# Attention in front of two MoE layers: another order of GpSimd's work and of SyncE's queue, fewer and smaller moves

## The reference

```python
def _attn_ref(q, k, v):                      # 4 batches x 8 heads, seq 576, head_dim 64
    scores = np.matmul(q, k.transpose(0, 1, 3, 2)) / np.sqrt(64)
    pos = np.arange(576)
    mask = (pos[:, None] // 64) >= (pos[None, :] // 64)
    scores = np.where(mask, scores, -1e9)
    attn = np.exp(scores - np.max(scores, axis=-1, keepdims=True))
    attn = attn / (np.sum(attn, axis=-1, keepdims=True) + 1e-09)
    return np.matmul(attn, v)
def _moe_ref(x, w_in, w_out):                # 2304 tokens, 512 -> 2048 -> 512
    h = x @ w_in
    return (h * np.clip(h + 3.0, 0.0, 6.0) / 6.0) @ w_out
def _moe2_ref(x, w_in, w_out):
    h = x @ w_in
    return (h * np.tanh(np.log1p(np.exp(h)))) @ w_out
```

## Time and profile before

| | us |
|---|---|
| median of 3 runs (984.53 to 993.46) | 988.69 |
| the profiled execution, its own time | 987.67 |
| its span | 985.9 |
| PE busy | 955.1 (97%) |
| PEld busy | 851.2 (86%) |
| DVE busy | 737.2 (75%) |
| ACT busy | 643.2 (65%) |
| POOL busy | 436.7 (44%) |

### The profile page before, as it was taken

One profiled execution on the slowest core, in us unless ns is written; L12 is line 12 of the kernel. 1 busy time (PEld: TensorE's weight loads), 2 busy tenths in 40 slices (PEclk: granted clock), 3 DMA queues, 4 the chain that ended last, 5 costly groups with the idle time before them and its releaser, 6 DMA issues.

```text
span 985.9 us, 17821 instructions
## 1 busy us (share of the span) xinstructions
PE 955.1 (97%) x6028; PEld 851.2 (86%) x6028; DVE 737.2 (75%) x1404; ACT 643.2 (65%) x1431; POOL 436.7 (44%) x423
## 2 busy tenths in 40 slices
PE   7898898999999999999999999999999999999998
PEld 6787787899888889988879898898988998998886
DVE  6777787867776576879797886877877777777654
ACT  6787898956544454454436557777777777776653
POOL 7787797776847496967775680000000000000000
PEclk9999999999999999999999999999999999999999
DMA  6878889765788977697777455556555654565255
GB/s 190 226 207 224 234 238 249 217 204 166 248 286 285 325 232 259 216 319 256 252 269 259 178 180 191 196 182 228 200 190 202 220 202 170 177 248 185 92 186 193
DMA packets 86330, 216.44 MB, mean 220 GB/s; under 512 B 10720, under 2 KB 17504, under 8 KB 86240
## 3 DMA queue, kind: packets, MB, share of 16 engines
q1 hardware_dynamic: 86096, 215.01, 66.7%
q10 hardware_dynamic: 144, 0.29, 0.1%
HBM read 162.07 MB, written 39.92 MB: 205 GB/s over the span
## 4 chain that ended last, share of the span: by engine, by line
PE 81%; DMA 6%; DVE 4%; SPq 3%; POOL 2%; issue 2%; ACT 1%; ACTq 0%; POOLq 0%; DVEq 0%
PE psum L1019 37%; PE psum L902 11%; PE psum L904 11%; PE psum L903 11%; PE psum L847 4%; DMA khi<-khi 4%; PE psum L826 3%; PE psum L806 2%; PE psum L807 1%; DVE ebuf L1591 1%; DMA ext_d<-ext_made 1%; POOL klo L1738 1%; SPq L557 1%; DVE ext_made L1497 1%; DVE glo L1597 1%
## 5 line engine op out<-in xcount | busy, mean ns | idle before, releaser
L1019 PE MATMUL psum<-ghi,osplit 128*128 128x512 f32 (+1 forms) x640 | 215.9, 371 | 0.0
L902 PE MATMUL psum<-xhi,whi 128*128 128x256 f32 (+1 forms) x640 | 187.4, 293 | 2.8 <-ACT snap L1238 2.7
L904 PE MATMUL psum<-xhi,wlo 128*128 128x256 f32 (+1 forms) x640 | 186.8, 292 | 0.0
L903 PE MATMUL psum<-xlo,whi 128*128 128x256 f32 (+1 forms) x640 | 186.6, 292 | 0.0
L1019 PE MATMUL psum<-osplit,ghi 128*128 128x512 f32 x576 | 180.8, 395 | 2.1 <-DVE glo L1597 1.3
L1597 DVE SCALAR_TENSOR_TENSOR glo<-ebuf,ghi 128x512 fp32r<-128x512 f32 x144 | 126.4, 878 | 26.2 <-ACT ghi L1286 18.3
L1286 ACT ACTIVATE ghi<-ebuf 128x512 fp32r<-128x512 f32 x144 | 90.3, 627 | 68.6 <-DVE ebuf L1591 37.7
L902 PEld LDWEIGHTS psum<-xhi,whi 128*128 128x128 f32 x640 | 120.8, 189 | 15.9 <-ACT snap L1238 4.3
L1882 POOL TENSOR_TENSOR osplit<-oraw,osplit 128x512 fp32r<-128x512 f32 x80 | 115.9, 1451 | 39.9 <-ACT osplit L1205 35.8
L1019 PEld LDWEIGHTS psum<-ghi,osplit 128*128 128x128 f32 x640 | 117.9, 189 | 15.8
L903 PEld LDWEIGHTS psum<-xlo,whi 128*128 128x128 f32 x640 | 120.8, 189 | 10.6
(11 more groups left out here) (118 smaller groups left out, 2142.8 us busy)
## 6 DMA issues: line engine op xcount, KB each, us to landing
ext<-ext_d SPq DMA_DIRECT2D x56, 768.0 KB, 4.4
osplit<-o_d SPq DMA_DIRECT2D x80, 512.0 KB, 5.7
oraw<-in_w_out SPq DMA_DIRECT2D x80, 256.0 KB, 5.6
wraw<-in_w_in SPq DMA_DIRECT2D x32, 512.0 KB, 5.4
ext_d<-ext_made SPq DMA_DIRECT2D x32, 384.0 KB, 5.3
attn_t<-ostage SPq DMA_DIRECT2D x64, 144.0 KB, 2.9
qkin<-in_qk SPq DMA_DIRECT2D x30, 288.0 KB, 4.5
o_d<-staged SPq DMA_DIRECT2D x32, 256.0 KB, 5.4
```

Of the source, the lines that this page charges most:

```text
L902: pe.matmul(dst, hi, xh, start=(start and cc == 0), stop=False, skip_group_check=True)
L903: pe.matmul(dst, hi, xl, start=False, stop=False, skip_group_check=True)
L904: last = pe.matmul(dst, lo, xh, start=False, stop=(stop and cc == 1), skip_group_check=True)
L1019: last = pe.matmul(bank(Y_BANK + c, n), stat, mov, start=(first and m == 0), stop=(final and m == 2), skip_group_check=True)
```

## The change

**GpSimd**: step n now begins with q and k of head n+4, then v of head n+2 (before: n+1), then the extra pieces. In the start, the lower part of head 1's q moves from GpSimd to DVE.

**DVE** takes over the weight sum of an early job (`mix_early`) and x's sum and scaling (`add_first_x`, `scale_first_x`), inside its step: sums between the row maxima of pieces 1 and 2, the scaling ahead of the row maximum of piece 3.

**PE**: the `klo` matmul uses rows 0 to 63 of `qs` and `klo` only. It leaves out the product of the two lower parts. `move_k_lo` is gone, and PE's wait for it.

**SP**: the output is stored by one DMA of 288 KB in place of two of 144 KB, into a DRAM tensor in another layout. A chunk of x now takes four DMAs in place of three: one of output and one of row-sum inverses for each half of the rows; this holds for all blocks of the first layer. An early weight load is two DMAs of 256 KB, one in a step. The order in a step is now `move_k_hi(n+3)`, `load_qk(n+6)`, extra loads (weights, x, w_out), `move_q_hi(n+4)`, `load_v(n+3)`, `store_o(n)`, `store_rinv`. The steps of the extra pieces change as in the tables.

```diff
-    lambda b: (12 if KIND[b] == SHORT else 6) if b < NBL else 1,
-    lambda b: 0 if KIND[b] == SHORT else 6 if b < NBL else 2 if b > NBL else 1)]
+    lambda b: (16 if KIND[b] == SHORT else 8) if b < NBL else 1,
+    lambda b: 0 if KIND[b] == SHORT else 8 if b < NBL else 2 if b > NBL else 1)]
...
-EARLY_JOBS = {3: 0, 7: 1, 11: 2, 26: 3}
-EARLY_X_LOAD, NEXT_X_LOAD = {10: (0,), 11: (1,), 12: (2,), 14: (3,)}, (27, 28)
-EARLY_X_ADD, EARLY_X_SCALE, EARLY_X_MIX = (16, 17, 18, 19), (17, 18, 19, 20), 21
-EARLY_X_HI, EARLY_X_LO = (22, 23, 24), (23, 24, 25)
-EARLY_LOADS = {0: 0, 3: 1, 8: 2, 20: 3, 22: 4, 29: 5}
+EARLY_JOBS = {3: 0, 6: 1, 9: 2, 12: 3}
+NEARLY, HALVED = len(EARLY_JOBS), 6
+EARLY_LOADS = {0: (0, 0), 1: (0, 1), 2: (1, 0), 3: (1, 1), 6: (2, 0), 7: (2, 1), 9: (3, 0), 10: (3, 1),
+               18: (4, 0), 19: (4, 1), 20: (5, 0), 21: (5, 1)}
+EARLY_X_LOAD, NEXT_X_LOAD = {11: 0, 13: 1, 15: 2, 16: 3}, (26, 27, 28, 29)
+EARLY_X_ADD, EARLY_X_MIX = (17, 18, 19, 20), 21
+EARLY_X_HI, EARLY_X_LO = (21, 22, 23), (22, 23, 24)
+EARLY_O_LOAD = (22, 23, 24)
...
@@ SP @@
-                for half in range(2):
-                    sp.dma_start(attn_t[half, head * DH:(head + 1) * DH, t0:t0 + SEQ],
-                                 ostage[n % OS][half * DH:(half + 1) * DH, :]).then_inc(o_stored[n % OS], 16)
+                sp.dma_start(attn_t[n % HEADS, :, t0:t0 + SEQ], ostage[n % OS][:, :]).then_inc(o_stored[n % OS], 16)
...
-            def load_x_chunk(x, c, cols, done):
-                sp.dma_start(x[:, 0:2, :], attn_t[:, c * P:(c + 1) * P, cols].rearrange("s p t -> p s t")
-                             ).then_inc(done, 16)
-                for h in range(2):
-                    sp.dma_start(x[h * DH:(h + 1) * DH, 2, :],
+            def load_x_chunk(x, c, cols, done, sides=range(2)):
+                for h in sides:
+                    rows = slice(h * DH, (h + 1) * DH)
+                    sp.dma_start(x[rows, 0:2, :],
+                                 attn_t[2 * c + h, :, cols].rearrange("(s d) t -> d s t", s=2)).then_inc(done, 16)
+                    sp.dma_start(x[rows, 2, :],
...
             for n in range(FIRST, NHEAD):
-                if n == FIRST or 0 <= n < NHEAD - 6:
-                    load_qk(n + 6)
-                if n == -1:
-                    move_k_hi(DIRECT)
-                    move_k_lo(DIRECT)
+                if DIRECT <= n + 3 < NHEAD:
+                    move_k_hi(n + 3)
+                if n == FIRST:
+                    load_qk(3)
+                elif n == FIRST + 1:
                     load_qk(4)
                     load_qk(5)
-                elif DIRECT < n + 3 < NHEAD:
-                    move_k_lo(n + 3)
-                    move_k_hi(n + 3)
+                elif 0 <= n < NHEAD - 6:
+                    load_qk(n + 6)
+                if n in EARLY_LOADS:
+                    load_w(*EARLY_LOADS[n])
+                if n in EARLY_X_LOAD:
+                    c = EARLY_X_LOAD[n]
+                    if c == 0:
+                        attention_stored(1)
+                    load_x_chunk(xst_plain[:, c, :, :], c, slice(0, HT), x_loaded[0])
+                if n in EARLY_O_LOAD:
+                    load_o(EARLY_O_LOAD.index(n))
...
@@ PE @@
-                    pe.wait_ge(k_lo_moved[n % QK], moves(n))
...
-                    last = pe.matmul(bank(pb, w), q_tile, klo[s][:, k0:k0 + w], start=False, stop=True)
+                    last = pe.matmul(bank(pb, w), q_upper, klo[s][0:DH, k0:k0 + w], start=False, stop=True)
...
@@ DVE @@
+                low = qs[1][DH:P, 0:SEQ]
+                dve.wait_ge(q_hi, 2)
+                nc.vector.tensor_tensor(low, qkin[1][DH:P, :], low.bitcast(F32), ALU.subtract
+                                        ).then_inc(direct_q_lo[1], 1)
...
+                if n in EARLY_JOBS:
+                    mix_early(EARLY_JOBS[n])
+                if n in EARLY_X_ADD:
+                    add_first_x(EARLY_X_ADD.index(n))
                 if in_use(n + 2):
                     row_max(n + 2, 2)
                 if in_use(n + 1):
                     split_probs_lo(n + 1, 1)
+                if n in EARLY_X_ADD:
+                    scale_first_x(EARLY_X_ADD.index(n))
...
@@ GpSimd @@
-                if DIRECT <= n + 4 <= QK:
+                if DIRECT <= n + 4 < NHEAD:
                     split_qk_hi(n + 4)
                     split_qk_lo(n + 4)
-                if n + 4 == DIRECT:
-                    split_second_k_lo()
-                    split_second_q_lo()
-                if DIRECT <= n + 4 <= QK:
+                    if n + 4 == DIRECT:
+                        split_second_k_lo()
                     place_q_lo(n + 4)
-                if in_use(n + 1):
-                    split_v_hi(n + 1)
-                    split_v_lo(n + 1)
+                if in_use(n + 2):
+                    split_v_hi(n + 2)
+                    split_v_lo(n + 2)
                 if n in EARLY_JOBS:
-                    mix_early(EARLY_JOBS[n])
                     split_early_hi(EARLY_JOBS[n])
...
-                if n in EARLY_X_ADD:
-                    add_x(0, EARLY_X_ADD.index(n))
-                if n in EARLY_X_SCALE:
-                    scale_x(0, EARLY_X_SCALE.index(n))
...
-                if QK < n + 4 < NHEAD:
-                    split_qk_hi(n + 4)
-                    split_qk_lo(n + 4)
-                    place_q_lo(n + 4)
```

More of the change, by code:

```diff
@@ L231, in own, with w_level @@
     return m - NEARLY
+def w_level(m):
+    return 16 * (m // 2 + 1 + min(m // 2 + 1, HALVED // 2))
 def moves(n):
@@ L336, in build @@
         k_hi_moved = [sem(f"k_hi_moved{s}") for s in range(QK)]
-        k_lo_moved = [sem(f"k_lo_moved{s}") for s in range(QK)]
         v_hi = sem("v_hi")
@@ L377, in build @@
         x_loaded = [sem(f"x_loaded{cc}") for cc in range(2)]
+        first_x_added = sem("first_x_added")
+        first_x_scaled = sem("first_x_scaled")
         x_added = sem("x_added")
@@ L572, in attention_stored, with load_w @@
                 sp.wait_ge(rinv_stored, 16 * NT * batches)
-            def load_w(m):
+            def load_w(m, half=None):
                 layer, p = JOBS[m][0:2]
@@ L582, in load_w @@
                     sp.wait_ge(ahead_lo, FT - 1 + m % 2)
-                sp.dma_start(wraw[m % 2][:, :], w_in[layer, p, :, :]).then_inc(w_loaded[m % 2], 16)
+                cols = slice(0, RES) if half is None else slice(half * RES // 2, (half + 1) * RES // 2)
+                sp.dma_start(wraw[m % 2][:, cols], w_in[layer, p, :, cols]).then_inc(w_loaded[m % 2], 16)
             def store_ext_hi(m):
@@ L729, in _ @@
                     store_rinv(n // HEADS)
-                if n in EARLY_LOADS:
-                    load_w(EARLY_LOADS[n])
-                for c in EARLY_X_LOAD.get(n, ()):
-                    if c == 0:
-                        attention_stored(1)
-                    load_x_chunk(xst_plain[:, c, :, :], c, slice(0, HT), x_loaded[0])
-                if n in (19, 20, 21):
-                    load_o(n - 19)
             for i in raw_at(-1)[0:2]:
@@ L1468, in attention_step, with mix_early, add_first_x, scale_first_x @@
                     split_probs_lo(n + 1, 1)
+                if n in EARLY_X_ADD:
+                    scale_first_x(EARLY_X_ADD.index(n))
                 if in_use(n + 2):
                     row_max(n + 2, 3)
+            def mix_early(m):
+                raw = wraw[m % 2]
+                a22, a21 = (raw[:, k * A_COLS:(k + 1) * A_COLS] for k in (2, 3))
+                dve.wait_ge(w_loaded[m % 2], w_level(m))
+                nc.vector.tensor_tensor(a21, a21, a22, ALU.add).then_inc(early_mixed, 1)
+            def add_first_x(k):
+                x = xst_plain[:, k, :, :]
+                dve.wait_ge(x_loaded[0], X_LOADS[0][1])
+                nc.vector.tensor_tensor(x[:, 0, :], x[:, 0, :], x[:, 1, :], ALU.add).then_inc(first_x_added, 1)
+            def scale_first_x(k):
+                x = xst_plain[:, k, :, :]
+                dve.wait_ge(first_x_added, k + 1)
+                nc.vector.tensor_tensor(x[:, 0, :], x[:, 0, :], x[:, 2, :], ALU.mult).then_inc(first_x_scaled, 1)
             def mix_w(m):
@@ L1803, in attention_step @@
                     scale_x(1, 2)
-            def mix_early(m):
-                raw = wraw[m % 2]
-                a22, a21 = (raw[:, k * A_COLS:(k + 1) * A_COLS] for k in (2, 3))
-                pool.wait_ge(w_loaded[m % 2], 16 * (m // 2 + 1))
-                nc.gpsimd.tensor_tensor(a21, a21, a22, ALU.add).then_inc(early_mixed, 1)
             def split_early_hi(m):
@@ L1844, in mix_x @@
                 k = KIND[blk]
-                if blk < NBL:
-                    pool.wait_ge(x_scaled, DC * blk + (DC if k == SHORT else 2 * cc + 2))
+                if blk == 0:
+                    pool.wait_ge(first_x_scaled, DC)
+                elif blk < NBL:
+                    pool.wait_ge(x_scaled, DC * (blk - 1) + 2 * cc + 2)
                 else:
```

56 lines of the change are left out of this document (20 added, 36 removed).

## The result

The change makes the kernel slower: 1034.34 us median of 4 runs (1032.69 to 1037.69), against 989.5 for the kernel before on the same chip (984.53 to 993.46, 4 runs). The ratio is 1.046, with a 95% interval of 1.0404 to 1.0516. The profiled execution took 1037.69 us, its span 1035.6.

The account below looks back on a forecast made before the run. PE was taken as the bound, with 19.1 us at most to win in the attention; 19.1 - 4.4 - 0.7 + 1.0 = 15.0, less 1.5, gives a gain of 13.5: median 975.2 us, range 967 to 988.

Parts of the forecast that it names:

- PE on 64 rows: Attention scores: a change of rows costs 0 to 0.02 us, 0 to 7.4 us over 31 steps; taken as 0.
- The cited rule: PE's weight loads: their time depends on columns, not rows, so the cost of 64 rows is exactly 0.
- The start: Head 1's scores wait less for q's lower part, now made by DVE: 1.0 us won, between -0.5 and 2.
- The attention's waits: PE's waits for k's upper part in the attention fall from 12.8 us to 4.4 us.
- the reserve: Attention: 1.5 us held back for steps that wait a little longer than the step-by-step count says.
- The landing of q's move: SP's queue in the attention: 3.9 us before, taken as 3.3 us without move_k_lo.
- The walk: Step-by-step lag of k's move: no PE wait before step 13, then waits in steps 13 to 24, 4.4 us together.
- some 4: Kernel before, steps 2, 5 and 10: the lowered clock adds some 4 us to PE's waits.
- long enough to have lowered the clock: Attention: none of PE's remaining waits reaches the 1.7 to 1.9 us of the three slow steps.
- The term of 0.7: Sums and scalings moved to DVE in the attention cost 0.7 us, between 0 and 4.
- The MoE part at 0: Two more DMA issues per block half, 1.2 us, lie inside SP's 311.6 us of waiting: cost 0.
- GpSimd's order at 0 to 1: Attention: taking q and k first on GpSimd is alone worth 0, up to 1 us.

Follow-up runs that it names:

- paired: The changed kernel with score tile 4's two pieces in the order khi, khi, klo, klo instead of khi, klo, khi, klo; 1020.37 us.
- rows128: The changed kernel with the klo matmul back on all 128 rows, still without the move of k's lower part; 981.26 us, ratio 0.9926.
- rows64_in_before: The kernel before with the klo matmul on rows 0 to 63 only, all moves and waits kept; 1025.70 us, ratio 1.0386.
- pool_order: no_move_in_before plus the change's GpSimd order (q and k of head n+4, then v of head n+2); 973.14 us, ratio 0.9882.
- old_layout: rows128 with the earlier output layout: two stores a head, three DMAs per chunk of x; 970.86 us, ratio 0.9864.
- early_x: old_layout with x's chunks loaded in steps 11 to 14 in place of 11, 13, 15 and 16; 973.14 us, ratio 0.9842.
- extras_last: rows128 with SP's extra loads issued behind store_o and store_rinv instead of ahead of move_q_hi; 979.86 us, ratio 0.9943.
- first_two_128: The changed kernel with the klo matmul on 128 rows for heads 0 and 1, 64 for the other 30; 1024.28 us, ratio 1.0387.
- no_move_in_before: The kernel before without move_k_lo and PE's wait for it, klo matmul still on 128 rows; 976.85 us, ratio 0.9899.

## Why the prediction was wrong

**The step that failed** is "PE on 64 rows": "A change of rows costs 0 to 0.02 ... I take 0". It measured 0.19 us where the load was hidden before (paired), 0.15 on average over eleven, 1.70 us a step, some 50 over the attention. My bound came from the wrong row. The 512-column matmul behind 64-row transposes is a change of rows, but in the kernel before that place is a change of kind as well, and such a change already costs 0.09 there: what a row change adds can't be read where the load is exposed anyhow. I also compared durations, whose ends are modelled, and not starts. The proper upper end was to be had from the same trace: all of a weight load, 0.19, uncovered at every change, which is 11 x 0.19 = 2.1 us a step. With it the upper end of the range would have gone from 988 to about 1050.

The kernel before even shows the effect itself, in PEld's timeline, which the prediction didn't read. Its only row changes are those into and out of the 64-row transposes:

```profile
127.45 0.38 PEld L826 LDWEIGHTS psum<-ident,prob 64*128 64x128 f32 x5 [0.25 <-issue]
127.90 0.19 PEld L806 LDWEIGHTS psum<-khi,qs 128*128 128x128 f32 x1
128.24 0.59 PEld L826 LDWEIGHTS psum<-ident,prob 128*128 128x128 f32 x4
```

The first two loads start together with their matmuls (127.45 and 127.90 in the earlier trace rows), so neither is hidden. The third is for transposes on 128 rows behind a matmul on 128 rows; it starts with that matmul (128.24), 0.23 us ahead of the transposes (128.47).

**The cited rule** on weight loads (the Trainium skill, TensorE: Matmul & The Clock Gate, LDWEIGHTS) agrees with the trace for the load itself: 0.183 us on 64 rows, 0.190 on 128. I took from it that the term is 0, which it doesn't say: it is about a load's length, not about what runs beside it. The Trainium skill, TensorE: Matmul & The Clock Gate, Part 2, says that a load is pulled ahead when row groups don't conflict or when it goes to the background buffer. Here 64 and 128 rows overlap in rows 0 to 63, and the load wasn't hidden (load and matmul both start at 130.24); with equal rows, which overlap more, it was (129.18 against 129.31). Which of the two conditions fails at a change of rows no run here shows.

**The start.** The term "1.0, between -0.5 and 2" is right where the rows are not in it: step 0 ended 1.3 us earlier in rows128. With the 64-row matmuls it was 7.5 late, by the clock. No rival had a clock that falls while PE is busy. The expectations put the half-clock stretch at 9.5 to 26 us; by the windows it is 9.7 to 26.8 and up to 1.0 us later in the other two kernels.

**The attention's waits.** In the changed kernel they are gone, because PE is slower: rows64_in_before, with the old order, has none either. rows128 is the kernel that this part of the prediction describes. It lost 11.3 us over 5.40 in steps 1 to 31 (0.5 of it is step 31's build), where the sum had 6.6 with the reserve; PE's waits for k were 7.9 us, not 4.4. The mechanism was right, the size off. The landing of q's move measured 3.8 us in the median, not 3.3: dropping `move_k_lo` didn't shorten it. That of k's move was 2.3; SP issues it after a wait for q's move, so less may stand ahead of it. The walk's clean steps 0 to 10 and stalls from 13 on came true (step 17: 7.47). The three half-clock stretches of the kernel before lasted 3.4 us each and so cost 5.1 us, an estimate, where the prediction has some 4. That no wait was "long enough to have lowered the clock" came true by luck: waits of 1.98 in rows128 and 2.06 in pool_order left the clock at 1.00, while a half-clock stretch followed those of 1.91 in the kernel before, 1.95 in old_layout and 1.89 in early_x.

**DVE.** In rows128 the weight sums took 0.42 to 1.12 us, x's sums 0.41 to 0.60 and the scalings 0.41 to 1.13. The scaling of 1.13 stood beside GpSimd's subtraction for v (from 135.13), those of 0.43 and 0.41 at 115.85 and 117.14 beside a GpSimd that waited for v, so not every sum takes the longer time. The term of 0.7 was small beside what I had not listed: DVE's wait for x, 1.2 us in rows128 and 3.1 in extras_last. I had named nobody who waits for the late x. A wait put in the middle of a full engine's order is paid by PE.

**The MoE part at 0** was wrong. "SP waits 311.6 us there" is a sum over the part; in the blocks where x is loaded the loads land late, and GpSimd waits for x, and PE now and then for GpSimd (1.8 us for `xlo` in rows128). GpSimd's wait for x rose from 24.4 us in the kernel before to 32.7. That term is 7 us, the difference of rows128 and old_layout.

**GpSimd's order at 0 to 1** is neither borne out nor refuted: 1.7 us by the ratios with SP's old order, within the noise, and 3.4 us less of PE's waits in the two traces, of which each is one execution.

## What to carry to other kernels

Fewer rows in a matmul saved nothing on PE here, and mixing them with full ones cost up to a weight load at each change, 0.19 us; group matmuls of equal rows, or leave harmless values in the other rows and run full. When a change brings a form that the trace doesn't show, bound it by what the pipeline could lose whole, here a whole weight load, not by the nearest row that looks like it, and look in PEld's timeline for loads that start together with their matmul. A queue of DMAs that waits for its own earlier DMA is a loop: everything between the two waits lengthens it. What stands behind the issue of the first is off the loop, but it comes later, and whoever waits for it must be looked up too.

## What was not expected of the hardware

With pairs of 128-row and 64-row matmuls from 7.5 us on, the granted clock fell at 9.7 to 10.7 us and stayed at 1.2 GHz for 17.1 us, in three kernels (changed, rows64_in_before, paired), though PE's records show no gap; with heads 0 and 1 on 128 rows it stayed at 2.4 GHz in first_two_128, and the same alternation later, over 200 us, never lowered it. Three kernels without a 64-row score (no_move_in_before, old_layout, early_x) also had a half-clock stretch in the start, but of 3.4 us. A move from SBUF to SBUF of 144 KB landed in 2.3 us in the median when SP had waited before issuing it (`move_k_hi` in rows128), and in 3.8 when it was issued straight behind a load of 288 KB or x's loads (`move_q_hi` there). In the changed kernel, where SP waited 29.9 us in all ahead of `move_q_hi`, that one landed in 2.5.
